# The state update of a chunked delta rule: one 48-column matmul written as a 32-column and a 16-column one

## The reference

```python
k_n = k / (np.linalg.norm(k, axis=-1, keepdims=True) + 1e-06)
state = np.zeros((B, H, D, D), dtype=np.float32)      # B, H, S, D = 4, 8, 768, 48
for t in range(S):
    kt, vt, bt = (k_n[:, :, t], v[:, :, t], beta[:, :, t, None])
    y[:, :, t] = np.einsum('bhd,bhde->bhe', q[:, :, t], state)
    v_old = np.einsum('bhde,bhd->bhe', state, kt)
    state = state + bt[:, :, :, None] * np.einsum('bhd,bhe->bhde', kt, vt - v_old)
```

## Time and profile before

| | before |
|---|---|
| median of 3 runs | 498.19 us (497.96 to 499.66) |
| the profiled execution, its own time | 498.19 us |
| its span, first to last instruction | 496.5 us |
| TensorE busy | 449.1 us (90%) |
| VectorE busy | 353.5 us (71%) |
| ScalarE busy | 304.1 us (61%) |
| mean granted TensorE clock, as a share of full speed | 0.997 |

### The profile page before, as it was taken

How to read it: one execution, slowest core, us unless ns; L and a number is a source line. 1 busy time by engine, 2 the same in 40 slices (tenths; PEclk the granted TensorE clock), 3 DMA queues, 4 the chain that set the end, 5 groups by cost and what they waited for, 6 DMA issues and landing times.

```text
span 496.5 us, 16832 instructions
## 1 busy us (share of the span) xinstructions
PE 449.1 (90%) x6916; PEld 332.9 (67%) x6916; DVE 353.5 (71%) x1171; ACT 304.1 (61%) x691; POOL 8.2 (2%) x20
## 2 busy tenths in 40 slices
PE   7658587978788899998999999999999999999997
PEld 5534465656566666664344788888888887887885
DVE  4998999999999998444622887565666655665662
ACT  2214488888888898775122777655656556556553
POOL 2000000000000000000000000000000000000000
PEclk9999899999999999999999999999999999999999
DMA  5901245666653434689999600100100100101001
GB/s 194 398 29 52 69 135 165 179 183 194 187 164 107 131 102 128 214 292 307 368 412 325 171 1 0 65 0 1 63 0 15 48 0 21 42 0 39 26 1 63
DMA packets 30565, 60.72 MB, mean 122 GB/s; under 512 B 3744, under 2 KB 12960, under 8 KB 30112
## 3 DMA queue, kind: packets, MB, share of 16 engines
q1 hardware_dynamic: 30496, 59.73, 36.5%
HBM read 53.43 MB, written 4.72 MB: 117 GB/s over the span
## 4 chain that ended last, share of the span: by engine, by line
PE 60%; DVE 28%; DMA 4%; issue 4%; ACT 3%; SPq 1%; DVEq 0%; ACTq 0%
PE bank L846 13%; PE bank L847 13%; PE bank L853 12%; DVE tmp L1146 9%; DVE tt L1151 8%; PE bank L815 4%; DMA win<-in_w_in 4%; PE bank L557 3%; DVE rr L1079 2%; PE bank L527 2%; DVE gt L1096 2%; PE bank L616 1%; PE bank L516 1%; DVE pd L1089 1%; DVE nv L1064 1%
## 5 line engine op out<-in xcount | busy, mean ns | idle before, releaser
L846 PE MATMUL bank<-g_h,wo_h 128*128 128x512 f32 x288 | 112.9, 392 | 0.1
L1353 DVE TENSOR_TENSOR g_l<-g,g_h 128x512 fp32r<-128x512 f32 x96 | 66.5, 693 | 64.5 <-ACT g_h L860 64.5
L847 PE MATMUL bank<-g_h,wo_l 128*128 128x512 f32 x288 | 112.1, 389 | 0.0
L860 ACT ACTIVATE g_h<-g 128x512 fp32r<-128x512 f32 x96 | 60.7, 632 | 69.2 <-DVE g L1348 69.1
L853 PE MATMUL bank<-g_l,wo_h 128*128 128x512 f32 x270 | 75.9, 389 | 0.0
L1348 DVE TENSOR_TENSOR g<-bank,sig 128x512 f32<-128x512 f32 x96 | 66.3, 690 | 13.3 <-ACT sig L1019 7.5
L860 ACT ACTIVATE zb<-bank 32x192 f32<-32x192 f32 x192 | 61.6, 321 | 19.9 <-PE bank L557 18.0
L1151 DVE TENSOR_TENSOR tt<-tt,tmp 128x126 f32<-128x126 f32 (+21 forms) x348 | 72.5, 251 | 0.0
L1146 DVE TENSOR_TENSOR tmp<-nm,tt 128x126 f32<-128x126 f32 (+21 forms) x348 | 72.1, 249 | 0.0
L1019 ACT ACTIVATE sig<-bank 128x512 f32<-128x512 f32 x96 | 57.2, 596 | 16.7 <-PE bank L815 16.4
L846 PEld LDWEIGHTS bank<-g_h,wo_h 128*128 128x128 f32 x288 | 54.0, 188 | 14.2 <-ACT res L860 2.6
(11 more groups left out here) (144 smaller groups left out, 443.2 us busy)
## 6 DMA issues: line engine op xcount, KB each, us to landing
slice<-in_w SPq DMA_DIRECT2D x48, 256.0 KB, 3.4
slice<-in_w SPq DMA_DIRECT2D x28, 384.0 KB, 7.0
kq<-in_kq_t SPq DMA_DIRECT2D x12, 512.0 KB, 6.5
kq<-in_kq_t SPq DMA_DIRECT2D x24, 256.0 KB, 2.9
vn<-in_v_nat SPq DMA_DIRECT2D x24, 192.0 KB, 3.3
out_t<-res SPq DMA_DIRECT2D x18, 256.0 KB, 2.0
kn<-in_k_nat SPq DMA_DIRECT2D x23, 192.0 KB, 2.8
win<-in_w_in SPq DMA_DIRECT2D x3, 1024.0 KB, 15.3
```

What stands on the lines that cost most here:

```text
L846: eng.matmul(acc[d][:], wo_h[:, f, cols], g_h[:, f % GR], start=(f == 0), stop=False)
L847: eng.matmul(acc[d][:], wo_l[:, f, cols], g_h[:, f % GR], start=False, stop=False)
L860: return eng.activation(out, src, ACT.Copy)
L1353: eng.tensor_tensor(g_l[:, f % GR], g[:, f % GR], g_h[:, f % GR].bitcast(F32), ALU.subtract).then_inc(s_gl, 1)
```

## The change

Each matmul of `update` is written as two. The first takes columns 0 to 31 of the keys and writes partitions 64a to 64a + 31 of the bank; the second takes columns 32 to 47 and writes partitions 64a + 32 to 64a + 47. The moving operand `zb` is the same for both and is passed twice. For each b the two 32-column matmuls (a = 0, 1) come first, then the two 16-column ones. The numbers computed are the same; waits and signals are the same.

```diff
                 for b in HALVES[half]:
-                    for a in range(2):
-                        g, at = 2 * b + a, HG * D * (b % 2)
-                        i = eng.matmul(sp[half][64 * a:64 * a + D, at:at + HG * D], kn[:, c % 3, g],
-                                       zb[:, g].rearrange("p q e -> p (q e)"), start=False, stop=True,
-                                       skip_group_check=True)
+                    for lo, hi in ((0, 32), (32, D)):
+                        for a in range(2):
+                            g, at = 2 * b + a, HG * D * (b % 2)
+                            i = eng.matmul(sp[half][64 * a + lo:64 * a + hi, at:at + HG * D], kn[:, c % 3, g, lo:hi],
+                                           zb[:, g].rearrange("p q e -> p (q e)"), start=False, stop=True,
+                                           skip_group_check=True)
                 i.then_inc(p_s, 1)
```

## The result

The changed kernel takes 502.26 us (median of 11 runs, 499.96 to 504.84) against 498.23 us of the kernel before beside it (11 runs, 497.66 to 500.03): a ratio of 1.0066, 95% interval 1.0039 to 1.0094. It is 4.0 us slower by the medians and 3.3 us by the ratio (2 to 5 us). The record has nine more executions of it, from 498.00 to 503.69 us; the median of all 20 is 502.2 us. The forecast was 498.1 us, within 497.0 to 499.9.

A forecast was written before the change was run, and what follows sets the result against it. VectorE was taken to bound the kernel until 171 us, then TensorE and ScalarE. From 498.19 us, matmuls 0, loads 0, change of form −0.1 and code 0 gave 498.1 us, range 497.0 to 499.9.

The forecast's parts named there:

- What bounds the kernel: Chunks 0 to 22: VectorE is the limit until 171 us, then TensorE and ScalarE; TensorE savings count only then.
- The split itself: In each update: 16 records cost 0.65 us of work like `pz`, as before; length difference taken as 0.
- its loads: In each update: eight weight loads become sixteen, hidden under the matmuls; cost 0.
- the change of form: After some updates, 0.12 to 0.14 us vanishes before 32-column groups; at most 0.42 us late, counted as 0.1.
- Code: TensorE's code queue: about 3 packets more, 0.4 of a stall; bounds −0.7 and +1.4 us, taken as 0.
- Covered stalls: TensorE's seven issue stalls: most covered, the 1.12 us at 105.63 by VectorE's chain; those at 175.63 and 226.74 nearly not.
- blocks: In updates, 32- and 16-column blocks don't run side by side: 0.65 us longer each, 506 us; chance 0.07.
- loads: In updates, sixteen loads stand in line with the matmuls: +0.76 us each, 508 us; chance 0.02.
- forms: In updates, 32 and 16 columns count as different forms: +1.05 us each, 522 us; chance 0.03.
- Code stalls on the chain: TensorE's code: two further stalls of 0.7 us on the chain, 499.6 us, no measurable change; chance 0.12.
- The gain passes: Shorter pitch comes through at all 14 late updates, stall at 226.74 falls elsewhere: 495.5 us; chance 0.05.
- TensorE idle on issue at new places of the last chunks: Sign in the last chunks that would show the forecast wrong through code stalls; no size given.

The follow-up runs named there:

- experiment 4: Changed kernel with the split only in chunks 0 to 13: 503.46 us; with the split only in chunks 14 to 22 (late split): 499.47 us.
- experiments 1 and 2: Kernel before, update matmuls split along the moving operand, 48 columns kept: 501.42 us; changed kernel without matmuls of columns 32 to 47: 498.02 us.
- experiment 6: Expert weights of the chunks loaded behind the last update, in both kernels: changed kernel 534.12 us, kernel before 532.54 us.
- experiment 7: Expert weights of chunks 4 to 19 loaded in quarters instead of halves: kernel before 499.56 us, changed kernel 503.99 us.

## Why the prediction was wrong

*What bounds the kernel.* Right as read, but not complete: a third limit, the supply of TensorE's code, was on average 0.6 us a chunk away from VectorE's pace, and no busy row shows it. It showed only in the seven "issue" rows.

*The split itself, its loads, the change of form.* Right: 0.84 us an update, the loads hidden, 0.11 to 0.14 us less ahead of groups of the same form. Of the at most 0.42 us, 0.21 came through; I had written that ScalarE lets 0.1 pass. The rule of the Trainium skill that was weighed ("TensorE: Matmul & The Clock Gate", Part 3, "The mechanism"; the section also lets a load go ahead into a background weight buffer, which the rule as quoted leaves out) would have had the sixteen loads in line, and by the loads' durations in the trace the group would have lasted over 1.7 us; it lasted 0.84, so for these forms the trace contradicts it.

*Code.* This is the step that failed. The mechanism and the amount were right (3 packets more), the size was not: taken at 0, bounded by +1.4, measured about +4.3 in the trace, less the small gain. I multiplied the additional packets by the share of packets that had stalled, 7 in 51, as if a stall were an accident of a packet. What counts is how fast the records use up a block, for every block of the stretch, not how many blocks were added. A chunk of 240 records uses 1.89 blocks where 1.76 are used before, and at 4.04 us a block that leaves 0.1 us under VectorE's pace on average where there were 0.6: between 60 and 230 us ten blocks came too late where five had. Six of the ten were covered; the four with a late packet made the 5.35 us at chunk 23. The rows to read it from were there: the stalls of before stand after records 2380, 2633, 3268, steps of 127, and the packets on the code queue could be timed.

*Covered stalls, and a term that is missing.* I wrote that most stalls are covered, because the 1.12 us at 105.63 were. The stall of 1.31 us at 145.19 in after is less than the slack of 1.47 and was not covered: the next `solve` came 1.35 us later than it would have (chunk 12 is 1.18 us behind, chunk 13 2.53). The prediction has no term for the clock. By the working above, stall and lower clock are 1.31 + 1.51 us together; less the 1.47 of slack that gives the 1.35. The same holds at chunk 5. That the clock is the part that decided there is worked out from the rows, not tested by a run; that stalls also lose time without it is shown by the late steps and by experiment 4.

*The rivals.* The three slower ones (blocks, loads, forms) are refuted by the pitch and by experiments 1 and 2. "Code stalls on the chain" is what happened, priced at 499.6 us and put among the cases of no measurable change with 0.12. "The gain passes" did not occur.

*The check list.* "TensorE idle on issue at new places of the last chunks" was the sign named for code; it is there at 192.18 and 223.80, and also in the early chunks, where I had not looked for it because VectorE sets the pace there.

*What stays open.* What sets the 4 us of a block. The 2.2 to 3.4 us from packet to restart are there whatever the variant; why a packet starts late behind its border, up to 4.5 us, is not shown. Fewer other transfers went with shorter stalls (experiment 6), shorter ones did not (experiment 7). Nor is it shown why the clock fell behind some stalls and not behind others as long, and how the 4 us divide between stalls and clock over many executions.

## What to carry to other kernels

Where a program is written out without loops and made of small matmuls, count the records between two stalls for "issue" and see whether they are multiples of one number; if they are, TensorE's code supply is a resource with a rate (here 127 matmul records and their loads in about 4 us), and every stretch can be put against it like any engine. Splitting a matmul is then not free even where the array and the loads hide it. A stall inside the slack is not free either, if the clock falls behind it: look at the granted clock of the stretch after each stall. The other way round, fewer and larger records might buy slack that no busy time shows; no run here tried it.

## What the runs showed that was not expected

The supply rate above: 14 blocks in 56.6 us with 272 records a chunk, stalled at nearly every border.

After some stalls TensorE's granted clock fell to the lower of its two levels, 1.2 GHz, for about 3 us. In after that was from 82.8 to 86.2 us, 0.6 us behind the end of the stall of 1.22, and from 147.6 to 151.0, 2.4 us behind the end of the stall of 1.31, while TensorE had been busy all the time in between. The update in the second stretch is long (timeline of TensorE):

```profile
147.49 1.43 PE L571 MATMUL bank<-zb,kn 128*32 128x192 f32 x16
```

Between 60 and 230 us every such stretch in the 14 traces begins within 3 us of the end of a stall of 1.1 to 2.0 us, or inside one. They are in the runs without added records too (experiments 2 and 7), and none is in before or experiment 4. Length alone doesn't decide: 1.86 us in experiment 4 and 1.90 at 223.80 in after had none behind them.

The clock rows of the first 40 us can't be read. They say 1.00 for the profiled executions of before and after and 0.64 for that of the late split (experiment 4):

```profile
0.00:30.00 30.00, 20.30 (x616) 15.15 (x619) 22.07 (x92) 7.42 (x13) 3.68 (x15) 0.64 0.71 256
```

But the same `ks` lasts as long in both, here in before and then in the late split, and 0.54 us at full clock:

```profile
30.94 0.87 PE L527 MATMUL bank<-state,kq 128*32 128x96 f32 x16
```

```profile
30.96 0.87 PE L527 MATMUL bank<-state,kq 128*32 128x96 f32 x16
```

So the lower clock was there in before as well; the records of the clock begin only at 40.6 us in its trace, and what has no record counts as full. The mean of 0.997 in the table of before leaves this opening out, and means above 0.975 and below it can't be compared. Among executions of one kind the mean does go with the time: of 35 executions of before above 0.975, the 25 at 0.992 or more average 498.3 us and the 10 below 500.2. The average of those 35 means is 0.993, of 17 of after 0.987. So the changed kernel spends more time at the lower clock than in one trace only.
